# First group of a fused convolution and MLP kernel: copies of activations moved from DMA to TensorE, first tiles reordered, sums on VectorE placed later

## What is computed

```python
w = softmax(weight_gen, axis=-1)                      # 7 taps per token and head, + 1e-9 in the sum
out[t] = sum(w[t, k] * x_pad[t + k] for k in range(7))# causal, per head: token t and the 6 before it
h = out @ w_in                                        # 192 -> 2048
g = where(h >= 1, h, where(h <= -1, 0, (h + 1)**2 / 4))
result = g @ w_out                                    # 2048 -> 192
```

## Time and profile before

| | |
|---|---|
| median of 3 runs | 1134.39 us (1134.28 to 1134.46) |
| profiled execution, its own time | 1134.3 us |
| its span | 1132.7 us |
| TensorE matmul busy | 1121.6 us, 99% of the span |
| VectorE / ScalarE / POOL busy | 790.6 / 878.6 / 810.8 us |
| share of TensorE in the chain that ended last | 96% |

### The profile page before, as it was taken

How to read it: one execution, slowest core, us unless ns; L and a number is a source line. 1 busy time by engine, 2 the same in 40 slices (tenths; PEclk the granted TensorE clock), 3 DMA queues, 4 the chain that set the end, 5 groups by cost and what they waited for, 6 DMA issues and landing times.

```text
span 1132.7 us, 28171 instructions
## 1 busy us (share of the span) xinstructions
PE 1121.6 (99%) x9790; PEld 926.0 (82%) x9790; DVE 790.6 (70%) x1280; ACT 878.6 (78%) x1655; POOL 810.8 (72%) x579
## 2 busy tenths in 40 slices
PE   8999999999999999999999999999999999999998
PEld 6888888888888888888888888888888888888886
DVE  6877667776677776677776777766777766777665
ACT  4887788777787877778777887877778778777775
POOL 6788887677876768867678876778767688676610
PEclk9999999999999999999999999999999999999999
DMA  7423334322334323344223343233442233442111
GB/s 155 101 46 62 69 69 79 74 54 44 69 74 79 60 51 60 65 79 79 56 37 70 74 79 65 54 52 67 77 79 58 45 66 67 79 79 51 19 47 29
DMA packets 287257, 74.15 MB, mean 65 GB/s; under 512 B 266304, under 2 KB 268352, under 8 KB 287232
## 3 DMA queue, kind: packets, MB, share of 16 engines
q1 hardware_dynamic: 280784, 72.92, 33.1%
q10 hardware_dynamic: 6448, 0.90, 0.6%
HBM read 24.10 MB, written 12.58 MB: 32 GB/s over the span
## 4 chain that ended last, share of the span: by engine, by line
PE 96%; DVE 2%; POOL 1%; ACT 1%; issue 0%; DMA 0%; DVEq 0%; ACTq 0%
PE slot L997 45%; PE acc_main L1023 30%; PE acc_rest L1034 20%; POOL taps_all L460 1%; DMA gen_in<-in_weight_gen 0%; DVE gate_low L813 0%; DVE conv L842 0%; DVE slot L807 0%; POOL in_low L584 0%; DVE taps_all L460 0%; DVE taps_all L842 0%; ACT xt_swap_high L704 0%; POOL out_w_main L592 0%; DVEq L91 0%; PE acc_rest L1044 0%
## 5 line engine op out<-in xcount | busy, mean ns | idle before, releaser
L1023 PE MATMUL acc_main<-gate_high,out_w_main 64*128 64x512 f32 x2032 | 623.0, 386 | 0.0
L813 DVE TENSOR_TENSOR gate_low<-slot,gate_high 128x512 fp32r<-128x512 f32 x510 | 352.8, 692 | 325.7 <-ACT gate_high L682 320.8
L671 ACT ACTIVATE half_relu<-slot 128x512 f32<-128x512 f32 x510 | 304.6, 597 | 185.2 <-PE slot L997 181.1
L1023 PEld LDWEIGHTS acc_main<-gate_high,out_w_main 64*128 64x128 f32 x2032 | 373.6, 184 | 40.0
L1023 PE MATMUL acc_main<-gate_low,out_w_main 64*128 64x512 f32 x1016 | 392.2, 386 | 0.0
L1034 PE MATMUL acc_rest<-gate_high,out_w_side 64*128 64x512 f32 x1016 | 392.2, 386 | 0.0
L1034 PE MATMUL acc_rest<-gate_low,out_w_side 64*128 64x512 f32 x1016 | 392.2, 386 | 0.0
L807 DVE SCALAR_TENSOR_TENSOR slot<-slot,square 128x512 f32<-128x512 f32 x510 | 350.4, 687 | 2.7 <-ACT square L677 2.7
L682 ACT ACTIVATE gate_high<-slot 128x512 fp32r<-128x512 f32 x510 | 303.5, 595 | 48.2 <-DVE slot L807 43.8
L677 ACT ACTIVATE square<-half_relu 128x512 f32<-128x512 f32 x512 | 322.8, 630 | 0.0
L460 POOL TENSOR_TENSOR taps_all<-x_in,tap_w 128x768 f32<-128x768 f32 x188 | 289.6, 1549 | 0.0
(11 more groups left out here) (140 smaller groups left out, 1810.0 us busy)
## 6 DMA issues: line engine op xcount, KB each, us to landing
x_in<-in_x SPq DMA_DIRECT2D x122, 132.0 KB, 3.0
out<-taps_all SPq DMA_DIRECT2D x189, 64.0 KB, 1.8
xt_side_high<-rest_turn SPq DMA_DIRECT2D x64, 128.0 KB, 3.1
xt_side_low<-rest_turn SPq DMA_DIRECT2D x64, 128.0 KB, 3.2
xt_swap_high<-xt_high SPq DMA_DIRECT2D x62, 128.0 KB, 2.5
xt_swap_low<-xt_low SPq DMA_DIRECT2D x62, 128.0 KB, 2.9
taps_all<-taps_all SPq DMA_DIRECT2D x31, 128.0 KB, 2.2
gen_in<-in_weight_gen SPq DMA_DIRECT2D x122, 28.0 KB, 1.9
```

The source lines that it names most:

```text
L671: nc.scalar.activation(half_relu[n % 2][:], tile_slot(pair, b, n)[:], ACT.Relu, scale=0.5, bias=0.5).then_inc(relu_done, 1)
L813: nc.vector.tensor_tensor(gate_low[n % GATES][:], tile_slot(pair, b, n)[:], gate_high[n % GATES][:].bitcast(F32), ALU.subtract).then_inc(g ...
L1023: ins = nc.tensor.matmul(acc_main[b][:], out_w_main[rows, n, 1 if j == 1 else 0, :], gate[rows, :], start=(turn == 0 and i == 0), stop=(tu ...
```

## The change

- ScalarE builds three 128x128 permutation matrices from the identity (six activations of 64 columns) ahead of `xt_high` of the first group. It makes the high part of input weights 2 before them, not later.
- TensorE multiplies `rest_turn` with the first two (into PSUM `slot[2]` and `slot[3]`) and `xt_low` with the third (into `acc_rest[1]`), as plain float32 products. ScalarE copies the first two results to `xt_side_high` and `xt_side_low`, VectorE the third to `xt_swap_low`. The four DMAs of the first group and the four subtractions are gone.
- TensorE runs tiles 0 and 1 through all nine units first, with the moves between them, then tiles 2 and 3, then 4 and 5. The four small products ahead of the first output unit are gone.
- The high part of out weights 0 goes from ScalarE to VectorE; out weights 1 go on ScalarE behind tile 2's square. VectorE forms the second group's tap weights behind the copies.
- The eight sums stand behind tiles 4 to 9 instead of 2 to 8; the turn of main and all behind it one tile later.

```diff
-HIGHS_AFTER = {2: ("in", 4), 3: ("in", 5), 5: ("out", 2), 6: ("in", 6), 7: ("in", 7), 9: ("out", 3)}
-
-
-SECOND_SUMS_AFTER = {2: ((0, 0),), 3: ((0, 1),), 4: ((0, 2),), 5: ((0, 3),), 6: ((1, 0),), 7: ((1, 1),),
-                     8: ((1, 2), (1, 3))}
+HIGHS_AFTER = {2: ("out", 1), 3: ("in", 4), 4: ("in", 5), 5: ("out", 2), 6: ("in", 6), 7: ("in", 7), 9: ("out", 3)}
+
+
+SECOND_SUMS_AFTER = {4: ((0, 0),), 5: ((0, 1),), 6: ((0, 2),), 7: ((0, 3),), 8: ((1, 0), (1, 1)), 9: ((1, 2), (1, 3))}
...
-FIRST_MAIN_AFTER, FIRST_REST_AFTER = (9, 9), (10, 10)
+FIRST_MAIN_AFTER, FIRST_REST_AFTER = (10, 9), (11, 10)
...
-FIRST_UNITS, FIRST_LAST_UNITS = (0, 1, 3, 4, 2, 6, 7), (5, 8)
-FIRST_FILLS = (4, 5)
+FIRST_FILLS = (0, 5)
...
+        moved_high, moved_low, moved_swap = slot[2], slot[3], acc_rest[1]
...
-            for q in range(QUADS // 2):
-                load_part(sp, 1, 0, q)
-            copy_side(sp, 0, 0, side_high_copied, xt_side_high, 0)
-            copy_side(sp, 0, 0, side_low_copied, xt_side_low, 1)
-            for q in range(QUADS // 2, QUADS):
+            for q in range(QUADS):
                 load_part(sp, 1, 0, q)
             for q in range(QUADS):
                 load_part(sp, 1, 1, q)
...
+        def high_rank(half):
+
+            return {1: 3, 2: 2}.get(half, half + 1)
...
+            def perm_columns(i):
+                for j in range(2):
+                    cols = slice(j * P // 2, (j + 1) * P // 2)
+                    src = ident[:, i:P:2] if i < 2 else ident[:, (1 - j) * P // 2:(2 - j) * P // 2]
+                    nc.scalar.activation(perms[:, i, cols], src, ACT.Copy).then_inc(perms_done, 1)
+
             in_high_part(0)
+            in_high_part(2)
+            act.wait_ge(ident_done, 2)
+            for i in range(3):
+                perm_columns(i)
             first_main_high(0)
             rest_high(0, 0)
             first_swap_high(0)
             first_main_high(1)
             first_swap_high(1)
             in_high_part(1)
+            act.wait_ge(first_side_moved, 1)
+            nc.scalar.activation(xt_side_high[0][:], moved_high[:], ACT.Copy).then_inc(side_high_copied, 32)
+            act.wait_ge(first_side_moved, 2)
+            nc.scalar.activation(xt_side_low[0][:], moved_low[:], ACT.Copy).then_inc(side_low_copied, 32)
             exponent(0, 1)
-            for half in range(2, EARLY_IN):
-                in_high_part(half)
-            for c in range(2):
-                out_high(c)
+            in_high_part(3)
...
+            dve.wait_ge(first_low_moved, 1)
+            nc.vector.tensor_copy(xt_swap_low[0][:], moved_swap[:]).then_inc(swap_low_copied, 32)
+            dve.wait_ge(out_w_loaded[0], 32)
+            nc.vector.tensor_copy(out_w_main[:, 0:CT, 0, :], out_raw[:, 0:CT, 0:P])
+            nc.vector.tensor_copy(out_w_side[:, 0:CT, 0, :], out_raw[:, 0:CT, P:D]).then_inc(out_high_done, 1)
             softmax(0, 1, "sum")
             softmax(0, 1, "inverse")
             tap_weights(dve, nc.vector, 0, 1)
-            for i in range(2):
-                for rows, other in ((LOWER, UPPER), (UPPER, LOWER)):
-                    nc.vector.tensor_tensor(first_columns(xt_swap_low[0], i)[rows, :], first_turned[i][other, :],
-                                            first_columns(xt_high[0], i)[other, :].bitcast(F32), ALU.subtract
-                                            ).then_inc(swap_low_copied, 8)
...
-            for j in FIRST_UNITS:
-                for n in range(FIRST_TILES):
+            def move(perm, src, to, moved):
+
+                nc.tensor.matmul(to[:], perms[:, perm, :], src, start=True, stop=True).then_inc(moved, 1)
+
+            def first_kind(tiles, j):
+                for n in tiles:
                     hidden_unit(0, 0, n, j)
-            for k in range(FIRST_TILES // 2):
-                for j in FIRST_LAST_UNITS:
-                    for n in (2 * k, 2 * k + 1):
-                        hidden_unit(0, 0, n, j)
-            for j in range(UNITS):
-                for n in (FIRST_TILES, FIRST_TILES + 1):
-                    hidden_unit(0, 0, n, j)
+
+            for j in (0, 1):
+                first_kind((0, 1), j)
+            pe.wait_ge(perms_done, 6)
+            pe.wait_ge(rest_turned, 1)
+            pe.wait_ge(main_turned, 1)
+            move(0, rest_turn[:], moved_high, first_side_moved)
+            move(1, rest_turn[:], moved_low, first_side_moved)
+            for j in (3, 4, 2):
+                first_kind((0, 1), j)
+            move(2, xt_low[0][:].bitcast(F32), moved_swap, first_low_moved)
+            for j in (6, 7, 5, 8):
+                first_kind((0, 1), j)
+            for k in (1, 2):
+                for j in range(UNITS):
+                    first_kind((2 * k, 2 * k + 1), j)
             for i in range(OUT_UNITS):
+                if i == 0:
+                    pe.wait_ge(taps_ready, 2)
                 if i in (0, OUT_MAINS // 2):
                     warm(FIRST_FILLS[i // (OUT_MAINS // 2)], acc_rest[0])
                 out_unit(0, 0, 0, 0, i)
```

More of the change, by code:

```diff
@@ L116, in build @@
         ident = sb("ident", [P, P])
+        perms = sb("perms", [P, 3, P])
         xt_high = [sb(f"xt_high{b}", [P, GT], F32R) for b in range(2)]
@@ L185, in build @@
         swap_low_copied = sem("swap_low_copied")
+        perms_done = sem("perms_done")
+        first_side_moved = sem("first_side_moved")
+        first_low_moved = sem("first_low_moved")
         side_high_copied = sem("side_high_copied")
@@ L582, in in_low_part @@
             parts, cols = in_columns(half)
-            eng.wait_ge(in_high_done, half + 1)
+            eng.wait_ge(in_high_done, high_rank(half))
             return ops.tensor_tensor(in_low[:, parts, cols], in_raw[:, parts, cols],
@@ L992, in hidden_unit @@
                 if first and n % CT == 0 and j in (0, 6):
-                    pe.wait_ge(in_high_done, 2 * (n // CT) + (2 if j == 6 else 1))
+                    pe.wait_ge(in_high_done, high_rank(2 * (n // CT) + (1 if j == 6 else 0)))
                 if first and n % CT == 0 and j in (1, 7):
```

## The result

The changed kernel takes 1137.76 us (median of 7 runs, 1137.39 to 1139.31) against 1134.39 (7 runs): 3.4 us more, a ratio of 1.0033 with a 95% interval of 1.0021 to 1.0045. The profiled execution took 1138.0 us round a span of 1136.1; before it was 1132.7. The forecast was 1137.0.

A forecast was written before the change was run, and what follows sets the result against it. TensorE, at full clock, bounds the kernel; only waits count. The marker unit going from 54.21 to 56.75 us gives 2.5, restart 0.1: 2.6 us on 1134.39, so 1137.0 us; range 1134.9 to 1139.4.

The forecast's parts named there:

- Bound and marker: TensorE at full clock, only waits count; marker unit: side-low unit of second group's first tile, at 54.21 us before.
- The moves: Three plain float32 products on TensorE, 0.87 us each, and four changes of unit mode, about 0.1 us each.
- First relu: End of tiles 0 and 1 at the start: first relu at 21.97 us against 22.06, worth 0.1 us.
- POOL, weights, fills: First group: POOL's taps 2 us late but ahead of the first sum, weights about when wanted, four fills less.
- Gate loop: ScalarE and VectorE in turn, tile 0's gate to tile 8's: left at 17.0 us.
- The moved sums: VectorE, two sums behind gate 8 and two behind gate 9: turn of main at 46.95 us, 2.8 us later.
- ScalarE: Behind the turn of main: gate_high, square, then exponent (0.28 us) ahead of second group's xt_high, at 48.36 us.
- Copies: Second group's eight SyncE copies behind xt_high: last issued at 53.6, landed at 56.7 us; TensorE waits 2.0 us.
- cheap moves: Rival on TensorE's moves: each takes a unit's 0.23 us, kernel 0.7 us slower, 1135.1 us; chance 0.15.
- dear moves: Rival ahead of first relu: moves of 1.7 us, overrunning permutations or slow PSUM copy; 1138 to 1140 us; chance 0.15.
- my chain: Main forecast, start through gates, sums, xt_high and copies to TensorE: 1137.0 us, own range 1136.4 to 1137.8; chance 0.65.
- the sums would not hold xt_high: Rival on second group's chain: xt_high keeps its old 45.87, copies are covered; 1133.5 to 1134 us; chance 0.05.

The follow-up runs named there:

- one move more: The changed kernel with the second move written twice, one more plain float32 product of 512 columns on TensorE: 1138.70 us.
- float32r moves: The changed kernel with its three moves as float32r products instead of plain float32, VectorE copying rest_turn once to a float32r tile: 1136.01 us.
- sums only: The kernel before with only the changed kernel's places of sums and turns, no moves on TensorE: 1137.14 us.
- mid sums: The changed kernel with the sums behind tiles 3 to 8 and the turns behind 9 and 10: 1135.68 us.
- exponent behind: The changed kernel with the second group's xt_high ahead of the third group's exponent on ScalarE: 1137.41 us.

## Why the prediction was right, and where its sizes were off

The sign, the mechanism and the place hold: the forecast was 2.6 us slower, it is 3.4, of which 3.1 in the span. Step by step:

- *Bound and marker.* Right for the span: the marker unit moved by 3.40 us and the span by 3.4; no wait of TensorE lies behind it. Wrong was that a shift found in the profile can be added to the median as it is. That put what lies outside the span at nothing, and it is 0.3 us.
- *Permutations on ScalarE.* Right, free: 0.99 us for six, in a gap.
- *The moves.* A size off, the largest one. A product's slot was put at 0.87 and is 0.86. What was too small is the change between half-row units and full-row products, put at 0.1 each way. It is four times 0.1: the last pair of units before a move takes 0.35 instead of 0.23 (16.79 to 17.14), the first product 0.96 instead of 0.86 (one move more, 16.90 to 17.86), the last product before the units again 0.95 (18.72 to 19.67 there), and the first pair of units 0.34 (17.77 to 18.11 in float32r moves); 0.4 a round trip, twice. From the first unit to VectorE's copy it is 21.19 - 16.48 = 4.7 us where 4.3 was forecast; of this, 0.1 lies between the end of the third move's record (19.96 + 1.13 = 21.09) and VectorE's start. The 0.08 us that I read off one row shows a part of the way out of unit mode only. The Trainium skill, TensorEngine Tiling (Array Packing), section Key Properties, says that a mode change drains the engine; 0.2 us a change agrees with it.
- *First relu.* Forecast 21.97, measured 22.70: 0.4 from the moves, and 0.33 because this execution had its first xt_high at 14.37 instead of 14.04. "Worth 0.1 us" was thus wrong in sign: the early finish of tiles 0 and 1 is a loss of 0.3 us, measured from the first xt_high in both (8.33 us against 8.02).
- *POOL, weights, fills.* Right. POOL's taps were 2.4 us later and in time, no weight was waited for.
- *Gate loop.* 17.0 taken, 40.94 - 24.00 = 16.94.
- *The moved sums.* Gate 8 to the turn of main: 6.68 forecast, 47.59 - 40.94 = 6.65. The new wait on low gate 9 is there: TensorE's start distance round it is 0.71 (46.42 to 47.13) instead of 0.23, so 0.5 us, not 0.8, since TensorE came to it later; the list shows 0.3 to 0.4 at each of two gates.
- *ScalarE.* Turn to xt_high: 1.41 forecast, 1.42.
- *Copies.* Right as the place. From xt_high's start to the marker unit 8.4 were forecast and 8.6 passed: the copies were issued a little faster, but the last landed after 3.48 us, outside the 3.0 to 3.2 of the earlier trace rows. In sums only and in mid sums it was 3.0 to 3.2 again, with float32r moves 3.3 to 3.6. Why it varies was not tried. The runs of a kernel spread most where TensorE waits for these copies (1.7 to 3.3 us between the lowest and the highest of changed, sums only, float32r moves and one move more, at most 1.0 where it doesn't wait), which fits a landing that varies; but exponent behind waits too and spreads by 0.6.

Together: the forecast 2.6, 0.4 more for the moves, 0.2 for the landing and 0.1 less in between are the 3.1 us of the spans. The other 0.3 lies outside them. It comes with the moves' part of the change and not with the places of the sums, since sums only doesn't have it; what takes it is open, as no trace shows what lies outside the span. The mechanism is shown by experiments, the moves' 0.4 by rows. The landing's 0.2 rests on single profiles.

Of the rivals, cheap moves fell by the rows. The kernel with float32r moves shows what they would have given, 1136.0 us and not 1135.1, since the changes of mode, the late landing and the 0.3 us outside the span stay. Of the dear moves 0.4 us came true, by the changes of mode and not by the products; 1137.76 lies just inside my chain's own 1136.4 to 1137.8. That the sums would not hold xt_high fell with sums only.

## What to carry to other kernels

Follow a delay past the engine that it is put on: here sums that were moved behind later tiles cost TensorE almost nothing where they stand (0.6 us of waits on low gates in sums only, 0.7 before), and 2.7 us ten microseconds later, through a turn, an activation and eight DMAs whose cover was half a microsecond. Before work is moved later in a startup, write down what is released by its last piece, and the cover of the last transfer in that chain. A copy of values that are rounded to float32r already need not be a plain float32 product: that alone took 1.75 us off the path. And a profile's span is not all of the time: look at the time less the span of every run before a shift in one is taken for a shift in the other.

## What the runs showed of the hardware

- A plain float32 product of 512 columns takes 0.86 us of TensorE from start to start (one move more, 17.86 to 18.72). For a float32r one 0.2 to 0.25 us is an estimate: two with the way back take 0.63 and one 0.43, less 0.2 for the change. The Trainium skill, FP8 and Floating Point Precision, section TensorE Precision Notes, gives four passes for true FP32; the ratio of the slots, about four, agrees.
- A round trip between 64-row units and 128-row products costs some 0.4 us, 0.1 at each of four places: the last pair of units, the first product, the last product and the first pair of units.
- ScalarE's copies of 64 columns, SBUF to SBUF, last 0.24 to 0.25 us each and start 0.15 us apart (six in 0.99); 0.27 for one was what scaling from longer ones gave.
- VectorE's cast of 512 columns from PSUM took 0.69 us. The one from SBUF took 0.42 us in the changed kernel, with POOL idle, and 0.62 to 0.64 in the four kernels with float32r moves, where it began while POOL was still at work. The other cast from SBUF in those kernels, with POOL idle, took 0.43.
- The time of an execution exceeds its span by 1.60 us in the kernel before and in sums only, and by 1.85 to 1.95 in all kernels with the moves.
